# First MLP in two halves of its hidden width, the first half between the attention steps

## The reference, cut to what matters

```python
def _attn_ref(q_l, k_l, v_l, q_g, k_g, v_g):           # B, H, Sl, D = 4, 8, 512, 64; Sg = 32
    s_g = scale * np.matmul(q_g, k_all.transpose(0, 1, 3, 2))      # 32 global queries see all keys
    out_g = np.matmul(sm(s_g), v_all)
    mask = np.abs(pos[:, None] - pos[None, :]) <= window           # window = 32
    s_l = np.concatenate([s_lg, np.where(mask, s_ll, -1e9)], axis=-1)
    out_l = np.matmul(sm(s_l), np.concatenate([v_g, v_l], axis=2))
    return np.concatenate([out_g, out_l], axis=2)

def _moe_ref(x, g_ln, w_ch1, w_ch2):                   # first MLP, 512 -> 2048 -> 512
    xn = (x - mu) / np.sqrt(var + 1e-06) * g_ln
    ch = np.maximum(xn @ w_ch1, 0.0) @ w_ch2
    return x + ch

def _moe2_ref(x, w_in, conv_w, w_out):                 # second MLP, 512 -> 1024 -> 512
    h = np.maximum(x @ w_in, 0.0)
    gate = 1.0 / (1.0 + np.exp(-conv_out))             # conv_out: 3-tap convolution of h over the tokens
    return h * gate @ w_out
```

## Time and profile before

| | |
|---|---|
| median of 3 runs | 830.81 us |
| the profiled execution | 830.24 us |
| its span, first to last instruction | 828.5 us |
| TensorE matmuls busy | 767.9 us, 93%, 7528 instructions |
| DVE busy | 426.3 us, 51% |
| ACT busy | 326.6 us, 39% |
| POOL busy | 316.8 us, 38% |
| granted TensorE clock, mean | 0.990 |
| moved by DMA | 80.85 MB |

### The profile page before, as it was taken

How to read it: one execution, slowest core, us unless ns; L and a number is a source line. 1 busy time by engine, 2 the same in 40 slices (tenths; PEclk the granted TensorE clock), 3 DMA queues, 4 the chain that set the end, 5 groups by cost and what they waited for, 6 DMA issues and landing times.

```text
span 828.5 us, 18608 instructions
## 1 busy us (share of the span) xinstructions
PE 767.9 (93%) x7528; PEld 751.9 (91%) x7528; DVE 426.3 (51%) x1057; ACT 326.6 (39%) x790; POOL 316.8 (38%) x281
## 2 busy tenths in 40 slices
PE   2698899778699999999999999999999999999997
PEld 2687888668699999999999999999999999999997
DVE  4599999898324322223112231212118777787774
ACT  4588888776344121111211112111424434444433
POOL 4888999859177001100101001000733334344332
PEclk9899999999999999999999999999999999999999
DMA  9867777831592241202421023200702011111000
GB/s 235 182 169 191 191 184 179 207 100 55 150 315 84 59 133 46 90 3 57 133 85 52 8 77 107 81 1 27 230 30 83 28 55 28 56 55 55 28 28 27
DMA packets 68229, 80.85 MB, mean 98 GB/s; under 512 B 14000, under 2 KB 54576, under 8 KB 68144
## 3 DMA queue, kind: packets, MB, share of 16 engines
q1 hardware_dynamic: 68144, 79.68, 34.5%
HBM read 57.36 MB, written 22.30 MB: 96 GB/s over the span
## 4 chain that ended last, share of the span: by engine, by line
PE 73%; DVE 14%; issue 3%; ACT 3%; SPq 2%; DMA 2%; POOL 1%; DVEq 0%; ACTq 0%; POOLq 0%
PE y_ps L462 32%; PE u_ps L462 32%; PE o_ps L462 4%; DVE p_lo L723 3%; DVE ln_nT L911 2%; DVE v_res L692 2%; DVE e_sb L708 2%; PE s_ps L462 1%; POOL h_lo L1211 1%; PE t_ps L495 1%; PE lx_ps L579 1%; PE ln_ps L581 1%; DVE v_end L699 1%; DMA kq_raw<-in_kqT 1%; SPq L345 1%
## 5 line engine op out<-in xcount | busy, mean ns | idle before, releaser
L462 PE MATMUL y_ps<-h_hi,w_hi 128*128 128x272 f32 x768 | 223.3, 291 | 7.0 <-POOL h_lo L1211 4.6
L462 PE MATMUL u_ps<-x_hi,w_hi 128*128 128x272 f32 (+1 forms) x768 | 223.3, 291 | 2.8 <-DVE x_lo L853 2.8
L462 PE MATMUL y_ps<-h_hi,w_lo 128*128 128x272 f32 x768 | 222.1, 289 | 0.0
L462 PE MATMUL u_ps<-x_lo,w_hi 128*128 128x272 f32 (+1 forms) x768 | 221.8, 289 | 0.0
L462 PE MATMUL u_ps<-x_hi,w_lo 128*128 128x272 f32 (+1 forms) x768 | 221.8, 289 | 0.0
L462 PE MATMUL y_ps<-h_lo,w_hi 128*128 128x272 f32 x768 | 221.7, 289 | 0.0
L859 DVE SCALAR_TENSOR_TENSOR h_lo<-u_ps,h_hi 128x272 fp32r<-128x272 f32 x128 | 56.5, 441 | 302.3 <-ACT h_hi L1044 302.3
L1044 ACT ACTIVATE h_hi<-u_ps 128x272 fp32r<-128x272 f32 x128 | 50.8, 397 | 291.8 <-PE u_ps L462 291.6
L462 PEld LDWEIGHTS y_ps<-h_hi,w_hi 128*128 128x128 f32 x768 | 145.2, 189 | 9.5 <-POOL h_lo L1211 6.8
L462 PEld LDWEIGHTS u_ps<-x_hi,w_hi 128*128 128x128 f32 x768 | 144.9, 189 | 2.9 <-DVE x_lo L853 2.9
L462 PEld LDWEIGHTS u_ps<-x_lo,w_hi 128*128 128x128 f32 x768 | 145.2, 189 | 0.0
(11 more groups left out here) (84 smaller groups left out, 1382.6 us busy)
## 6 DMA issues: line engine op xcount, KB each, us to landing
kq_raw<-in_kqT SPq DMA_DIRECT2D x64, 280.0 KB, 5.2
w_raw<-in_wall SPq DMA_DIRECT2D x24, 512.0 KB, 5.0
v_raw<-in_vx SPq DMA_DIRECT2D x32, 260.0 KB, 5.7
c_raw<-y_cols SPq DMA_DIRECT2D x8, 548.0 KB, 4.0
c_res<-x_cols SPq DMA_DIRECT2D x8, 544.0 KB, 5.6
y_cols<-y_sb SPq DMA_DIRECT2D x8, 544.0 KB, 4.8
out_T<-y_sb SPq DMA_DIRECT2D x8, 544.0 KB, 3.4
x_rows<-x_loc SPq DMA_DIRECT2D x32, 128.0 KB, 1.8
```

The costliest lines, as they stand in the source:

```text
L462: return nc.tensor.matmul(out, lhsT, rhs, start=start, stop=stop, **kw)
```

## The change

The three stages are put on one list of steps, the same for all engines (`END` = 194 of them). Attention is steps 0 to 66. From step 22 on each step also has one unit of the first MLP: 64 units with the first 8 tiles of the hidden width, in chunks of two tiles of 128 tokens (the last of three), then 40 with the other 8 tiles, in chunks of three or four. Tokens go in tiles of 128 over batches, with the 32 global tokens of all four batches in a tile of their own: 17 tiles, 2176 tokens. The second MLP starts at step 126.

- The attention output stays in SBUF (`x_loc`, `x_g`), is normalised there and transposed straight into its high and low parts (`xn`), which the first half uses and which are also stored for the second half (`xn_parts`, `xb`). The weights take in g_ln (four scalings of 128 columns a tile on ACT), and the 8 tiles in SBUF are overwritten by those of the second MLP.
- `down` now has the hidden tile as the stationary operand and 512 columns of weights as the moving one, so its result is rows. The first half's result goes to memory (`y_first`) and is loaded again in the second half, where POOL adds x and DVE the second half's result; that is transposed, split and stored (`y_parts`).
- Scores of the global queries are done once a group, 16 matmuls of 320 columns, in the banks of `y_ps` and from the third group on in those of the scores. Global values alternate between the four heads.
- Raw keys and queries have two slots instead of four and 1280 columns instead of 1120; keys lie in memory in the order of use, so that one copy of 736 columns replaces three. Exponents are four activations of 128 columns a step instead of two of 224. The last part of the values is POOL's for every head.
- Transposes and outputs have one PSUM bank each, after step 18 and output 8; before that two.
- The zero tokens are 1024 elements a DMA instead of 512.

The core of the diff; the rest moves the loops of the other engines onto the same steps.

```diff
+U0 = 22
+CH1 = [tuple(range(2 * c, 2 * c + 2)) for c in range(7)] + [(14, 15, GT)]
+CH2 = [(14, 15, GT), (0, 1, 2), (3, 4, 5), (6, 7, 8, 9), (10, 11, 12, 13)]
+N1, N2 = HALF * len(CH1), HALF * len(CH2)
+C0 = U0 + N1 + N2
+CUNITS = 2 * BATCH * FT2
+END = C0 + CUNITS + 4
+Y_ORDER = [t for chunk in CH2 for t in chunk]
...
+def unit(n):
+
+    if n < N1:
+        return n // HALF, CH1[n // HALF], n % HALF
+    return (n - N1) // HALF, CH2[(n - N1) // HALF], HALF + n % HALF
+
+
+def ln_step(t):
+    return 72 if t == GT else 16 * (t // QT + 1) + 4 + t % QT
...
+T_BANK = [k % 2 if T_STEP[k] < 19 else 0 for k in range(len(T_SEQ))]
...
+def o_bank(k):
+    return k % 2 if k <= O_FLIP else 0
...
+W_STEP = [6 + 3 * j for j in range(8)] + [68 + 2 * j for j in range(8)] + [U0 + N1 + 4 + 2 * j for j in range(8)]
...
-        kq_raw = [sb(a, f"kq_raw{r}", [P, KR + S], f32) for r in range(4)]
+        kq_raw = [sb(a, f"kq_raw{r}", [P, KQW]) for r in range(2)]
...
+            def load_head(m):
+                if m == 2:
+                    sp.wait_ge(klo0_ok, 1)
+                if m >= 2:
+                    sp.wait_ge(qglo_ok, m - 1)
+                sp.dma_start(kq_raw[m % 2][0:D, :], kqT[m]).then_inc(kq_in[m % 2], 16)
+                sp.dma_start(kq_raw[m % 2][D:P, :], kqT[m]).then_inc(kq_in[m % 2], 16)
...
+                if j >= 2:
+                    sp.wait_ge(wlo_ok, j - 1)
+                sp.dma_start(w_raw[j % 2][:, :], wall[j]).then_inc(w_in[j % 2], 16)
+
+            def w_load_step(j):
+                return (4 if j < 2 else W_STEP[j - 2] + 1)
...
+                chunks = [(s0, c, QT + c) for c in range(4)] + [(s1, 0, 0)]
+                for i, (slot, c, vc) in enumerate(chunks):
+                    for n, (pp, vn) in enumerate(PARTS):
+                        for hh in range(GH):
+                            last = mm(bank[SG * hh:SG * (hh + 1), 0:DV],
+                                      (p_hi, p_lo)[pp][slot][:, P * c + SG * hh:P * c + SG * (hh + 1)],
+                                      v_parts(GH * G + hh)[vn][:, DV * vc:DV * (vc + 1)],
+                                      i == 0 and n == 0, i == 4 and n == 4)
...
+            def up(n):
+                c, tiles, f = unit(n)
+                width = P * len(tiles)
+                if n < N1 and f == 0:
+                    pe.wait_ge(tlo_ok, max(T_IDX[("LN", t)] for t in tiles) + 1)
+                if n < HALF:
+                    pe.wait_ge(wlo_ok, n + 1)
+                if N1 <= n < N1 + HALF:
+                    pe.wait_ge(wlo_ok, f + 1)
+                if n >= N1 and f == HALF and c >= 1:
+                    pe.wait_ge(xb_in[(c - 1) % 2], 16 * sum(len(CH2[k]) for k in range(1, c + 1) if (k - c) % 2 == 0))
                 if n == 0:
+                    pe.wait_ge(o_ok, O_FLIP)
+                elif n == 1:
+                    pe.wait_ge(tlo_ok, T_LAST_U1 + 1)
+                else:
+                    pe.wait_ge(hlo_ok, n - 1)
+                x = x_chunk(n)
                 for k in range(KT):
+                    for i, (w, part) in enumerate(((w_hi, 0), (w_hi, 1), (w_lo, 0))):
+                        last = mm(u_ps[n % 2][:, 0:width], w[f][:, P * k:P * (k + 1)],
+                                  x[:, KT * part + k, 0:width], k == 0 and i == 0, k == KT - 1 and i == 2)
+                last.then_inc(up_ok, 1)
...
+            def down(n):
+                c, tiles, f = unit(n)
+                pe.wait_ge(hlo_ok, n + 1)
+                hi, lo = h_parts(n)
+                first, final = f % HALF == 0, f % HALF == HALF - 1
+                for j in range(len(tiles)):
+                    if first:
+                        if n < N1:
+                            if c > 0:
+                                if j < 2:
+                                    pe.wait_ge(ev_ok, after_chunk1(c - 1) + j + 1)
+                        elif c == 0:
+                            pe.wait_ge(ev_ok, after_chunk1(7) + j + 1)
+                        elif j < len(CH2[c - 1]):
+                            pe.wait_ge(ya_ok, after_chunk2(c - 1) + j + 1)
+                    for i, (h, w) in enumerate(((hi, w_hi), (lo, w_hi), (hi, w_lo))):
+                        last = mm(yb[j], h[:, P * j:P * (j + 1)], w[f][:, DM:2 * DM], first and i == 0, final and i == 2)
+                    last.then_inc(dn_ok, 1)
...
+            for s in range(END):
+                G = burst_in(s)
+                late = G is not None and G >= 2
+                if s < PAIRS and not late:
+                    scores(s)
+                if G is not None:
+                    global_scores(G)
+                if 0 <= s - 2 < PAIRS:
+                    transposes(s - 2)
+                if global_values_in(s) is not None:
+                    global_values(global_values_in(s))
+                if 0 <= s - U0 < N1 + N2:
+                    up(s - U0)
+                if 0 <= s - C0 < CUNITS:
+                    up_c(s - C0)
+                for use in extras(s):
+                    extra_transposes(use)
+                if s < PAIRS and late:
+                    scores(s)
+                if 0 <= s - 3 < PAIRS:
+                    values(s - 3)
+                if 0 <= s - 1 - U0 < N1 + N2:
+                    down(s - 1 - U0)
...
+                if j < 2 * HALF:
+                    for k in range(KT):
+                        last = nc.scalar.mul(raw[:, P * k:P * (k + 1)], raw[:, P * k:P * (k + 1)], g_sb[:, k:k + 1])
+                    last.then_inc(wg_ok, 1)
+                    act.wait_ge(wg_ok, j + 1)
+                at = j if j < 2 * HALF else j - 2 * HALF
+                nc.scalar.copy(w_hi[at][:, :], raw[:, :]).then_inc(whi_ok, 1)
```

More of the change, by code:

```diff
@@ new lines, in values_of, with o_head, o_group, o_before @@
+def values_of(use):
+    return V_IDX[("T", use[1])] if use[0] == "T" else V_IDX[("G", use[1])]
+def o_head(m):
+    return m + m // GH
+def o_group(G):
+    return 5 * G + 4
+O_FLIP = 8
+def o_bank(k):
+    return k % 2 if k <= O_FLIP else 0
+def o_before(k):
+    return k - 2 if k <= O_FLIP else k - 1
+DN = [0]
+for _n in range(N1 + N2):
+    DN.append(DN[-1] + len(unit(_n)[1]))
+def after_chunk1(c):
+    return sum(map(len, CH1[:c]))
+def after_chunk2(k):
+    return sum(map(len, CH2[:k]))
+def stats_before(b):
+    return 9 * b
@@ new lines, in x_chunk, with x_tile, h_parts @@
+        def x_chunk(n):
+            c, tiles, _ = unit(n)
+            if n < N1:
+                return xl if c == len(CH1) - 1 else xn[c % 2]
+            return xl if c == 0 else xb[(c - 1) % 2]
+        def x_tile(t):
+            c = next(c for c in range(len(CH1)) if t in CH1[c])
+            at = P * CH1[c].index(t)
+            return c, (xl if c == len(CH1) - 1 else xn[c % 2])[:, :, at:at + P]
+        def h_parts(n):
+            r, width = n % HSLOTS, P * len(unit(n)[1])
+            if n < N1 - HALF:
+                return h_hi[r][:, 0:width], h_lo[r][:, 0:width]
+            return hb[r][:, 0, 0:width], hb[r][:, 1, 0:width]
@@ new lines, in transposed, with transposes @@
+            def transposed(use, blocks):
+                k = T_IDX[use]
+                if T_BEFORE[k] >= 0:
+                    pe.wait_ge(tlo_ok, T_BEFORE[k] + 1)
+                for c, src in enumerate(blocks):
+                    last = nc.tensor.transpose(t_ps[T_BANK[k]][:, P * c:P * (c + 1)], src, identf[:, :])
+                last.then_inc(t_ok, 1)
+            def transposes(gp):
+                pe.wait_ge(exp_ok, gp + 1)
+                transposed(("T", gp), [e_sb[gp % 2][:, P * c:P * (c + 1)] for c in range(4)])
@@ L676, in _ @@
+            for r in range(HEADS):
                 v.memset(qg_st[r][:, :].bitcast(f32), 0.0)
[L677 to L682 removed]
@@ L1214, in batch_c @@
[L1214 to L1225 removed]
+                n = 1 if b == BATCH else QT
```

1733 lines of the change are left out of this document (771 added, 962 removed).

## The result

The changed kernel takes **852.1 us** (median of 4 runs, 851.8 to 854.5) where the kernel before, on the same chip, takes 831.1: a ratio of 1.025, with an interval of 1.022 to 1.029. The forecast was 812 and the range ended at 838, so the change is slower where I gave that 0.18. The profiled execution, the slowest of the four, has a span of 852.6 us; the sum had 810.5. So 42.1 us are to be explained.

A forecast was written before the change was run, and what follows sets the result against it. Attention was taken as bound by DVE and its neighbours, the MLPs by TensorE's columns. 103.5 us to step 22, 236, 40, 33, 195.7, second MLP 198 and end 4.4 gave 810.5; plus 1.7 for the execution, 812 us, range 786 to 838.

The forecast's parts named there:

- less the 4.6 of waits for POOL: Second MLP: 201.7 us less 4.6 of waits for POOL's chunk roundings, 1 us kept for result tiles, 198 us.
- The start: Up to step 7: first weight tile and head 6 queue behind zero-token stores, ACT waits; 43.5 us, ends 40 and 54.
- I take 4.0: Steps 7 to 21, attention alone: 4.0 us a step, 60 us for 15 steps, ends 51 and 69.
- The ring: Attention-only steps: two raw-key slots make a load wait for POOL's low query two heads before; 4.2 us a step.
- Steps 22 to 65: Attention and first MLP together: 5.36 us a step, 236 us for 44 steps, ends 5.0 and 5.8.
- The waits I listed: Steps 22 to 65, per 8 steps: TensorE waits at global values 0.6, global scores 0.4, layer-norm 2.5 every 16 steps; 2.2 us.
- The last heads: Steps 66 to 77: 12 units 33.5 us, layer-norm tiles 2.2, last heads 1.5, one wait 3; 40 us.
- The second half: First MLP's second half: matmuls 185.4 us, 17 transposed result tiles 7.3, bank hand-overs 3, ending at 608 us.
- All widths: TensorE matmuls at full clock: 256 columns 0.12 us, 384 columns 0.173, 512 columns 0.226.
- the 825 rival: First MLP: 512 columns take 0.238 us, nothing saved on width, and a slow start; 825 us, chance 0.17.
- The rival of the shared banks: Steps 22 to 65: shared transpose and output banks bind, 6.1 us a step, 33 us more; 845 us, chance 0.18.
- my signs of being wrong: Groups over 46 us apart with p_lo or x_loc waits; 512-wide at 238 ns; first up after 115 us; xb or yl waits.

The follow-up runs named there:

- Experiment 1: Changed kernel with ACT's copy of a finished second-MLP output out of its bank one step earlier: 839.0 us, 1.011 of the kernel before.
- experiment 2: Changed kernel with the eight zero-token stores issued at step 30 instead of step 4: 838.3 us, 1.011 of the kernel before.
- POOL's order: Edit: POOL makes the query's low half before the weights' low half and the value residue; alone on the changed kernel 838.5 us, 1.009 of the kernel before.
- Experiment 11: Changed kernel with zero tokens at step 30, earlier output copy, and no scaling of first-MLP weights on ACT: 819.0 us, 0.987 of the kernel before.
- experiment 3: Changed kernel with the second half's residual loads issued earlier and POOL's add one step behind them: 850.4 us, 1.025 of the kernel before.
- kernel 9: Changed kernel with zero tokens at step 30, the earlier output copy and POOL's order: 818.2 us, 0.984 of the kernel before.
- the two cures alone: Changed kernel with zero tokens at step 30 and the second MLP's output copy one step earlier: 828.9 us, 0.9964 of the kernel before.
- a weight table that was too late: Both cures, earlier residual loads with later add, first eight weight tiles at steps 15 to 28: 829.7 us; with POOL's order 828.1 us.

## Why the prediction was wrong

**The steps that failed.** Three, in waits and in the time of a step that is all waiting, and none in the work.

*The second MLP, 201.7 "less the 4.6 of waits for POOL": a term was missing.* I added 1 us for the result tiles and left the hand-over of its output bank at what it had been. The change had put ACT's copy (`read_o`) one step later relative to the first down of the next chunk. Experiment 1 gives it 12.7 us of the 17.2 missed. The other 4.4 are the last downs and four transposed tiles of the first MLP, which the forecast had counted before step 126: without the hand-overs the stage takes 206.8 us, and 202.4 + 4.4 is that.

*"The start", 43.5 us with 54 as its upper end.* Mechanism right: zero tokens ahead of the weight tile, ACT waiting in order. The size was off. Step 7 began at 32.5 and the wait fell in step 8, 14.3 us for ACT, so step 9 began at 55.1, where the forecast's own pace gives 43.5 + 8 = 51.5. Moving the stores took 13.4 us off. I had counted on the time the stores took before and some of it hidden; nothing was, as ACT stood in front of both the exponents and the keys, and the tile landed late besides. That the miss is only 3.6 us is luck, for two errors stand against each other: with nothing but the stores moved (experiment 2) step 9 begins at 41.7, where the forecast had 48 with the wait hidden (40 + 8), so the pace up to there was 6.3 too slow, and the wait, 13.4 instead of 3.5, was 9.9 too short.

*"I take 4.0" for a pure step.* Measured 4.65 (60.5 us for steps 9 to 21), 8.5 us missed. The ring I described binds there for a good part: with POOL's order a step takes 4.28 us (55.6/13) and ACT's waits for raw keys are gone. Experiment 11 agrees, but would also if ACT's work alone were the limit. I had worked out 4.2 from the ring and took less, "as part of the ring's time runs beside a step that is late anyway". It doesn't. Taking 4.2 would have won back only 2.6 of the 8.5 us: the measured step is over both sums (ring 4.2, ACT alone 3.4). I read this as a loop through ACT and POOL whose members also do the step's other work in order, which takes more than its own sum. (That sum also had a weight tile at 2.05 us on ACT, where my own prices give 1.05 + 4 x 0.30 = 2.25 and the trace 2.3.) A second term stood at nothing: every matmul was priced at full clock, and TensorE had 0.81 of it from 55.1 to 115.6 us (0.95 from 31 to 94 us in the kernel before). How the rest divides between the two is open. The order inside a step on POOL stood in the code, and I used it to size the loop without seeing that it could be turned round.

The rest is small. Steps 22 to 65 came to 5.48 us each against 5.36, within its ends. The waits I listed are there, and as long in sum as I had them (13 us against 12), but of another kind; these are TensorE's two longest from 115 to 357 us:

```profile
PE t_ps L544 <- DVE p_lo L739: 6.3, 5, 1.7
PE t_ps L544 <- DVE ln_n L809: 2.8, 2, 1.4
```

The first is transposes waiting for the one bank, which is free when DVE has read p_lo out of it. Most of the rest is work: a step with a layer-norm tile takes 5.13 us where a plain one takes 4.44, 0.69 more where I had 0.43 for its transposes. The last heads, 4.7 us over, had the one wait I priced (2.8 us at step 68) and one of 1.1 at step 72; behind the first TensorE was at 1.2 GHz from 369.1 to 372.5 us, where six downs took 2.7 us instead of 1.4. The second half, 5.2 us over for the same work, holds the stall of 5.8 (experiment 3).

**What was right.** All widths, within about 2%. Two places in the changed kernel, in order of time:

```profile
402.99 0.33 PE L502 MATMUL u_ps<-xl,w_lo 128*128 128x384 f32 x1
403.16 0.51 PE L502 MATMUL u_ps<-xl,w_hi 128*128 128x384 f32 x2
403.51 0.33 PE L502 MATMUL u_ps<-xl,w_lo 128*128 128x384 f32 x1
403.68 0.39 PE L502 MATMUL y_ps<-w_hi,h_hi 128*128 128x512 f32 x1
403.91 0.40 PE L502 MATMUL y_ps<-w_hi,h_lo 128*128 128x512 f32 x1
404.14 0.40 PE L502 MATMUL y_ps<-w_lo,h_hi 128*128 128x512 f32 x1
```

384 columns start 0.173 us apart and 512 columns 0.23, near the 0.173 and 0.226 priced, and the eight units of 384 take 33.0 us, as forecast. That rules out the 825 rival's 0.238. The rule of the Trainium skill (TensorE: Matmul & The Clock Gate, Back-to-back issue gap), N / 2.4 + 2.5 ns, disagrees here as well: it would have 216 ns at 512 columns.

The rival of the shared banks had the right sign and nearly the right time, 845, for the wrong reason: it wanted 6.1 us a combined step, 33 us in all, and the steps came to 5.48. Its mechanism is seen, the 6.3 us of waits for the one transpose bank, but the 42 us arose elsewhere. Of my signs of being wrong two came: the first up matmul after 115 us, and waits behind the loads of x and of the first half's result in the second half. ACT's prices held too: exponents of 128 columns 0.40 and 0.39 us (forecast 0.40), the key copy 0.80 (0.81), four scalings 1.28 (1.2). ACT was the busiest engine from step 7 to 21, as said, and had the waits for w_raw and the keys.

**What the change is worth.** With its waits mended (kernel 9) it is 1.6% faster than the kernel before, and 1.4% faster than that kernel with the same cure for its zero tokens (0.984/0.998). In its trace the second MLP takes 206.7 us, as in experiment 1 (206.8), and stage 22 to 65 238.8. The forecast of 812 was near what the idea can give (818); what it had not priced is what the new order did to the hand-overs. Kernel 9 is not the kernel that was forecast, though: its order on POOL is a further change, and the two cures alone stand at 0.4% faster.

## What to carry to other kernels

When work is interleaved in a fixed order, list for every buffer which instruction frees it and what stands ahead of that instruction on its engine; a copy-out or a low-half split that slips behind one tile of unrelated work costs its full wait each time it comes round (12.7 us for seven bank copies, 10 us for a raw slot). Don't average a loop's time with the busiest engine's: take the loop, and take it as the least it can be. A short wait of TensorE can cost again through its clock: look at the granted clock behind it. And test cures alone and on a clean base: POOL's order was worth 0.2% beside a weight table that was too late, and 1.2% without it.

## What was unexpected of the hardware

- Global values of four heads that alternate between column groups run far closer than I took: 100 matmuls of 65 columns in 0.96 us (147.04 to 148.00), a median of 6 ns from start to start, against 1.5 us forecast and 2.92 before. In order of time, the first of them and the matmul behind the last:

```profile
147.04 0.21 PE L502 MATMUL o_ps<-v_raw,p_hi 128*32 128x65 bf16 x4
147.08 0.25 PE L502 MATMUL o_ps<-v_res,p_hi 128*32 128x65 bf16 x8
147.15 0.21 PE L502 MATMUL o_ps<-v_raw,p_lo 128*32 128x65 bf16 x4
...
148.00 0.51 PE L502 MATMUL u_ps<-xn,w_hi 128*128 128x256 f32 x2
```

  The Trainium skill (TensorE: Matmul & The Clock Gate, Part 3, The mechanism) draws matmuls at different tile positions of the array starting some 4 ns apart; the trace agrees in kind, at 6 ns between column groups. The estimate that the prediction made from that page, some 0.75 us for the 100, was nearer than my 1.5.
- Eight stores of 1024 4-byte elements each hold SP's queue together for 8.8 us (30.97 to 39.80), 0.6 to 2.25 us an issue, where a load of 512 KB is issued in 0.7.
- A load of 256 KB (x rows, issued at 497.48 us, between stores of transposed results) took 13.0 us to land, where the median of its 17 is 5.9. Four stores of the global tile's transposed result had been issued before it and took 14.6 us to land (median). Between 490 and 515 us the DMA engines were busy nearly throughout at only 143 GB/s, with most packets small:

```profile
DMA packets 5214, 3.57 MB, mean 143 GB/s; under 512 B 3093, under 2 KB 4189, under 8 KB 5213
```
